# Masking, maximum and shift of the local scores in PSUM, and the sums of v behind the normalisations of the pair before

## What is computed

```python
q_d = q.reshape(B, H, Sd, factor, D).mean(axis=3)      # k_d and v_d likewise; factor 4
out_up = np.repeat(sm_attn(q_d, k_d, v_d), factor, axis=2)
mask = np.abs(pos[:, None] - pos[None, :]) < factor
scores = np.where(mask, scale * np.matmul(q, k.transpose(0, 1, 3, 2)), -1000000000.0)
scores = scores - np.max(scores, axis=-1, keepdims=True)
attn = np.exp(scores)
attn = attn / (np.sum(attn, axis=-1, keepdims=True) + 1e-09)
x = out_up + np.matmul(attn, v)                        # heads side by side: (2304, 512)
h = x @ w_in;  x = np.maximum(0.01 * h, h) @ w_out
h = x @ w_in2; out = (h - np.tanh(h)) @ w_out2
```

## Time and profile before

| what | value |
|---|---|
| median of three runs | 975.33 us |
| lowest, highest | 973.02, 978.2 us |
| the profiled execution: time, span | 974.49, 972.7 us |
| TensorE matmuls busy | 948.7 us (98% of the span) |
| VectorE, ScalarE, GpSimd busy | 553.2, 560.7, 406.8 us |
| chain that ended last: TensorE, GpSimd, ScalarE, VectorE | 82%, 6%, 4%, 2% of the span |

### The profile page before, as it was taken

How to read it: one execution, slowest core, us unless ns; L and a number is a source line. 1 busy time by engine, 2 the same in 40 slices (tenths; PEclk the granted TensorE clock), 3 DMA queues, 4 the chain that set the end, 5 groups by cost and what they waited for, 6 DMA issues and landing times.

```text
span 972.7 us, 19772 instructions
## 1 busy us (share of the span) xinstructions
PE 948.7 (98%) x6960; PEld 889.8 (91%) x6960; DVE 553.2 (57%) x1074; ACT 560.7 (58%) x1355; POOL 406.8 (42%) x343
## 2 busy tenths in 40 slices
PE   6898999999999999999999999999999999999998
PEld 5688999999999999999999989899899899898997
DVE  5853563555445534544334566876676666766764
ACT  4555644645546455445354777775576665766654
POOL 3554823625517337245161847623233233233232
PEclk9979999999999999999999999999999999999999
DMA  6861322112111210212001302100000000000000
GB/s 134 202 193 44 100 51 51 27 25 50 30 39 31 50 31 19 49 27 66 1 2 48 94 24 87 33 34 1 11 22 1 32 0 0 32 0 0 33 1 33
DMA packets 87797, 41.48 MB, mean 43 GB/s; under 512 B 60352, under 2 KB 81344, under 8 KB 87744
## 3 DMA queue, kind: packets, MB, share of 16 engines
q1 hardware_dynamic: 87744, 40.78, 16.0%
HBM read 36.04 MB, written 4.72 MB: 42 GB/s over the span
## 4 chain that ended last, share of the span: by engine, by line
PE 82%; POOL 6%; ACT 4%; issue 3%; DVE 2%; SPq 2%; DMA 1%; POOLq 0%; ACTq 0%; DVEq 0%
PE ph L514 12%; PE ph L515 12%; PE ph L516 12%; PE acc L590 6%; PE acc L591 6%; PE acc L543 6%; PE acc L592 6%; PE acc L544 6%; PE acc L545 6%; PE banks L412 2%; PE banks L431 2%; PE banks L444 2%; POOL in_lo L1071 1%; POOL g_lo L1092 1%; PE banks L405 1%
## 5 line engine op out<-in xcount | busy, mean ns | idle before, releaser
L1092 POOL TENSOR_TENSOR g_lo<-scratch,g_hi 128x384 fp32r<-128x384 f32 x96 | 126.0, 1312 | 257.3 <-ACT g_hi L705 257.1
L940 DVE TENSOR_TENSOR ph<-g,ph 128x288 f32<-128x288 f32 x128 | 59.0, 461 | 165.7 <-ACT g L719 165.1
L514 PE MATMUL ph<-x_hi,w_hi_a 128*128 128x288 f32 (+1 forms) x448 | 144.6, 323 | 0.9 <-DVE g_lo L927 0.7
L515 PE MATMUL ph<-x_lo,w_hi_a 128*128 128x288 f32 (+1 forms) x448 | 140.8, 314 | 0.0
L516 PE MATMUL ph<-x_hi,w_lo_a 128*128 128x288 f32 (+1 forms) x448 | 140.7, 314 | 0.0
L1071 POOL TENSOR_TENSOR in_lo<-w_whole,in_hi 128x512 fp32r<-128x512 f32 x64 | 84.8, 1325 | 131.8 <-ACT in_hi L685 131.8
L719 ACT ACTIVATE g<-ph 128x288 f32<-128x288 f32 x128 | 52.6, 411 | 132.8 <-PE ph L516 132.8
L1076 POOL TENSOR_TENSOR out_lo<-w_whole,out_hi 128x512 fp32r<-128x512 f32 x64 | 86.3, 1348 | 71.9 <-ACT out_hi L689 71.8
L974 DVE SCALAR_TENSOR_TENSOR scratch<-scratch,ph 128x384 f32<-128x384 f32 x96 | 53.2, 554 | 109.7 <-ACT scratch L768 105.1
L767 ACT ACTIVATE scratch<-ph 128x384 f32<-128x384 f32 x96 | 46.8, 488 | 108.3 <-PE ph L516 106.8
L927 DVE TENSOR_TENSOR g_lo<-ph,g_hi 128x288 fp32r<-128x288 f32 x128 | 58.6, 458 | 59.2 <-ACT g_hi L705 59.2
(11 more groups left out here) (265 smaller groups left out, 2681.7 us busy)
## 6 DMA issues: line engine op xcount, KB each, us to landing
out_dram<-o_stage SPq DMA_DIRECT2D x18, 256.0 KB, 2.0
w_whole<-in_moe_w_in_dram SPq DMA_DIRECT2D x16, 256.0 KB, 3.9
w_whole<-in_moe_w_out_dram SPq DMA_DIRECT2D x16, 256.0 KB, 4.4
qn<-in_q_dram SPq DMA_DIRECT2D x26, 144.0 KB
kn<-in_k_dram SPq DMA_DIRECT2D x26, 144.0 KB
v4n<-in_v_dram SPq DMA_DIRECT2D x26, 144.0 KB
vw<-in_v_dram SPq DMA_DIRECT2D x26, 122.5 KB
scratch<-in_moe_w_in_dram SPq DMA_DIRECT2D x8, 256.0 KB, 2.9
```

The lines of the kernel that those rows point to most:

```text
L514: pe.matmul(bank, whi, x_hi[:, c, 0:width], start=(c == 0), stop=False)
L515: pe.matmul(bank, whi, x_lo[:, c, 0:width], start=False, stop=False)
L940: dve.tensor_tensor(ph1[:, f % 2, 0:T1], g1[:, f % 2, :], ph1[:, f % 2, 0:T1], ALU.max)\
L1092: pool.tensor_tensor(g2_lo[:, f % 3, :], g2[:, f % 2, :], g2_hi[:, f % 3, :].bitcast(F32), ALU.subtract).then_inc(g_lo_done, 1)
```

## The change

Two things are changed. In the first batch GpSimd's sums of v move from step 4 to step 6 of a pair; with the stagger of four slots and the order inside a slot they then stand behind step 10 of the pair before. In the twelve later pairs (i > 0) VectorE masks the local scores where they lie in PSUM, takes the maximum of each half from there, and writes `pl` only with the subtraction, for each half by itself. Bank 0 is free after the first half's subtraction, bank 1 after the second's, and ScalarE's exponential waits for the latter. The first four pairs keep the old way. TensorE's instructions are as before.

```diff
+        def first_of(i):
+
+            return isinstance(i, int) and i == 0
...
                 elif step == 7:
-                    act.wait_ge(s.sub_l, i + 1)
+                    if first_of(i):
+                        act.wait_ge(s.sub_l, 1)
+                    else:
+                        act.wait_ge(s.bank_free[1], uses1(i, 3))
                     act.activation(s.pl[:, :, :], s.pl[:, :, :], ACT.Exp, scale=L_SCALE).then_inc(s.exp_l, 1)
...
+            def local_scores(s, bank):
+                n0, n1 = (0, NBA) if bank == 0 else (NBA, NB)
+                return s.banks[:, bank, 0:(n1 - n0) * WIN].rearrange("p (n w) -> p n w", w=WIN)
+
+            def maxima(s, n0, n1):
+                return s.mxl[:, n0:n1].rearrange("p (n o) -> p n o", o=1).to_broadcast([P, n1 - n0, WIN])
...
                 elif step == 4:
                     dve.wait_ge(s.bank_full[0], uses0(i, 3))
-                    src = s.banks[:, 0, 0:NBA * WIN].rearrange("p (n w) -> p n w", w=WIN)
-                    dve.tensor_tensor(s.pl[:, 0:NBA, :], src, band[:, 0:NBA, :], ALU.add).then_inc(s.bank_free[0], 1)
+                    half = local_scores(s, 0)
+                    if first_of(i):
+                        dve.tensor_tensor(s.pl[:, 0:NBA, :], half, band[:, 0:NBA, :], ALU.add)\
+                            .then_inc(s.bank_free[0], 1)
+                    else:
+                        dve.tensor_tensor(half, half, band[:, 0:NBA, :], ALU.add).then_inc(s.masked_half, 1)
                     dve.tensor_reduce(s.kdT[:, :], s.kT[:, PAD:PAD + S].rearrange("p (t f) -> p t f", f=FACTOR),
                                       AX_X, ALU.add).then_inc(s.means_done, 1)
+                    if not first_of(i):
+                        dve.wait_ge(s.masked_half, 2 * i - 1)
+                        dve.tensor_reduce(s.mxl[:, 0:NBA], half, AX_X, ALU.max).then_inc(s.max_half, 1)
...
                 elif step == 5:
                     dve.wait_ge(s.bank_full[1], uses1(i, 3))
-                    src = s.banks[:, 1, 0:(NB - NBA) * WIN].rearrange("p (n w) -> p n w", w=WIN)
-                    dve.tensor_tensor(s.pl[:, NBA:NB, :], src, band[:, NBA:NB, :], ALU.add).then_inc(s.bank_free[1], 1)
-                    dve.wait_ge(s.bank_free[1], uses1(i, 3))
-                    dve.tensor_reduce(s.mxl[:, :], s.pl[:, :, :], AX_X, ALU.max).then_inc(s.max_l, 1)
-                    dve.wait_ge(s.max_l, i + 1)
-                    dve.tensor_tensor(s.pl[:, :, :], s.pl[:, :, :],
-                                      s.mxl[:, :].rearrange("p (n o) -> p n o", o=1).to_broadcast([P, NB, WIN]),
-                                      ALU.subtract).then_inc(s.sub_l, 1)
+                    half = local_scores(s, 1)
+                    dve.tensor_tensor(half, half, band[:, NBA:NB, :], ALU.add).then_inc(s.masked_half, 1)
+                    dve.wait_ge(s.max_half, 2 * i - 1)
+                    dve.tensor_tensor(s.pl[:, 0:NBA, :], local_scores(s, 0), maxima(s, 0, NBA), ALU.subtract)\
+                        .then_inc(s.bank_free[0], 1)
+                    dve.wait_ge(s.masked_half, 2 * i)
+                    dve.tensor_reduce(s.mxl[:, NBA:NB], half, AX_X, ALU.max).then_inc(s.max_half, 1)
+                    dve.wait_ge(s.max_half, 2 * i)
+                    dve.tensor_tensor(s.pl[:, NBA:NB, :], half, maxima(s, NBA, NB), ALU.subtract)\
+                        .then_inc(s.bank_free[1], 1)
...
             def attention(step, s, i):
-                if step == (4 if isinstance(i, int) and i == 0 else 5):
+                if step == (6 if first_of(i) else 5):
```

More of the change, by code:

```diff
@@ L165, in __init__ @@
                 self.v_loaded = sem(f"v_loaded_{which}")
+                self.masked_half, self.max_half = sem(f"masked_half_{which}"), sem(f"max_half_{which}")
                 self.max_l, self.max_d = sem(f"max_l_{which}"), sem(f"max_d_{which}")
@@ L875, in attention @@
                     dve.tensor_reduce(s.kdT[:, :], s.kT[:, PAD:PAD + S].rearrange("p (t f) -> p t f", f=FACTOR),
                                       AX_X, ALU.add).then_inc(s.means_done, 1)
+                    if not first_of(i):
+                        dve.wait_ge(s.masked_half, 2 * i - 1)
+                        dve.tensor_reduce(s.mxl[:, 0:NBA], half, AX_X, ALU.max).then_inc(s.max_half, 1)
+                elif step == 5 and first_of(i):
+                    dve.wait_ge(s.bank_full[1], uses1(i, 3))
+                    dve.tensor_tensor(s.pl[:, NBA:NB, :], local_scores(s, 1), band[:, NBA:NB, :], ALU.add)\
+                        .then_inc(s.bank_free[1], 1)
+                    dve.wait_ge(s.bank_free[1], uses1(i, 3))
+                    dve.tensor_reduce(s.mxl[:, :], s.pl[:, :, :], AX_X, ALU.max).then_inc(s.max_l, 1)
+                    dve.wait_ge(s.max_l, 1)
+                    dve.tensor_tensor(s.pl[:, :, :], s.pl[:, :, :], maxima(s, 0, NB), ALU.subtract)\
+                        .then_inc(s.sub_l, 1)
```

## The result

The changed kernel takes 967.24 us, the median of nine runs (962.71 to 968.43), against 976.53 (972.22 to 981.4) of the kernel before in nine runs beside it. The ratio is 0.9899, 95% interval 0.987 to 0.9929. The forecast was 968.0. Two executions of the kernel before, 981.0 and 981.19 us in one of those series, were in a slower state and are left out of its mean.

What follows compares the result with a forecast made beforehand. TensorE was taken to carry almost the whole 972.7 us span, so only its idle or low-clock time could pay. 974.49 - 2.4 (first batch) - 4.2 (tile 0) + 0 (banks) = 967.9, forecast 968.0 us, range 964.0 to 972.5.

Steps and rivals of the forecast that it cites:

- the forecast's two terms: The gains summed: -2.4 us from GpSimd's order in the first batch, -4.2 us from the subtraction in tile 0.
- The first batch, -2.4 us: A's normalisation no longer waits behind B's v sums on GpSimd; layer one starts 2.4 us earlier, from -1.9 to -3.
- Tile 0, -4.2 us: First pair: subtraction no longer stands behind GpSimd; transposes start 2.9 us earlier, clock gives 0.75 and 0.6; from 0 to -4.9.
- Banks held longer, 0: Later pairs free PSUM banks only after the subtraction; at most 0.1 us in five first pairs; term 0, from +0.5 to -0.5.
- The price of the new instructions: VectorE in later pairs: 0.43 us for 280 elements, 0.51 for 350, a PSUM operand costing nothing extra.
- The clock ahead of layer one: Rival: TensorE's fall to the 1.2 GHz level from 47.8 to 61.4 us doesn't come; time 964 us; 13%.
- my sum: The whole kernel: 974.49 - 2.4 - 4.2 = 967.9 us, forecast 968.0.
- my terms without clock: The first batch's and tile 0's gains, leaving out the 0.75 and 0.6 us expected from tile 0's clock.
- The subtraction doesn't stand behind GpSimd: Rival denied here: in tile 0 the subtraction still stands, only the first term is left, 972.1 us; 10%.
- the first batch's gain was not eaten: Rival denied here: a load of C or D, or D's normalisation behind its v sums, eats it; 970.3 us; 10%.
- PSUM operands cost nothing more: Rival denied here: later pairs' six PSUM instructions cost more than neighbours show; 969.9 us at 0.05 each, 979.4 at 0.22; 7%.

Runs made afterwards that it cites:

- after again: The changed kernel unedited, run once more beside other kernels: 967.09 us, ratio 0.9897 to the kernel before.
- the clock held: Ten dummy transposes of the identity added on TensorE, in the first batch and ahead of layer one; on the changed kernel 962.33 us, on the kernel before 967.46.
- the subtraction late: Kernel before with v sums at step 6 and ten dummy transposes, plus a small extra VectorE maximum ahead of the maximum of tile 0's first pair: 966.12 us.
- the kernel with halves: The changed kernel with masks writing `pl` in SBUF and maxima and subtractions reading it there: 977.09 us; with ten dummy transposes 974.12.
- the order alone: Kernel before with only the first batch's v sums moved to step 6: 967.5 us; with ten dummy transposes 965.67.
- PSUM alone: Changed kernel with the first batch's v sums back at step 4: 970.97 us; with ten dummy transposes 966.5.
- both once more: The changed kernel with the ten dummy transposes, run again beside other kernels on the same chip: 963.46 us, ratio 0.9887 to the kernel before.

## Why the prediction was right, point by point

**The time.** That 968.0 lies so near 967.24 is in part luck. The sum had 6.6 us of gain, counted from 974.49 us; between the medians there are 9.3, counted from 976.53. The gain was put 2.7 us too small and the start 2.0 us too low, and the two nearly cancel. Two profiles that both have the fall of the clock ahead of layer one, before and after again, differ by 7.4 us: 3.20 up to layer one, 0.64 from there to the scores, 3.84 in the stretch, and 0.3 given back behind it. That is the forecast's two terms and 0.8 us more.

**The first batch, -2.4 us.** The mechanism was right, the term a little small: 2.75 us at C's scores as stepped (2.7), but 3.0 at layer one. I had taken 0.3 off for ScalarE's queue; in its place there is a gain of 0.24, since B's normalisation stood behind C's sums as well. I had not looked whether the pattern that I had found for A came again for B.

**Tile 0, -4.2 us, of which 1.35 of clock.** The stretch got shorter by 3.83 us in the profiles (21.37 to 17.54): 2.46 up to the first transpose, where I had 2.9, and 1.37 behind it for the clock, where I had 1.35. With the clock held the standstill costs 2.88 up to the first transpose (16.33 and 13.45, with the subtraction late and without) and nothing behind it; it is longer there because GpSimd's split began 5.58 us behind the scores, in the kernel before 5.17. The remaining wait is 1.11 where I said 0.65: TensorE gets there 12.34 us after the scores (66.22 less 53.88), as stepped (12.38), but ScalarE's weight copy came 0.4 us later than stepped, 8.66 us behind the scores instead of 8.28. What I had not seen is that the standstill need not be there. In the kernel before it was decided by 0.01 us (the expectation of the last kernel says 0.04), and in both profiles with the old subtraction and the clock held it went the other way without any edit to the subtraction. In how many runs of the kernel before it comes is not known, since only one was profiled.

**Banks held longer, 0.** Right: 0.1 us in each later tile, as a gain. The price of the new instructions was right too, 444 to 526 ns against 0.43 to 0.51 us forecast, the mask over 350 elements, which writes in place, being the dearest. By an estimate from the table of the Trainium skill that I had weighed, "VectorE: DVE Perf Modes", section "The TRN2 errata", a PSUM input costs some 65 ns more. The subtraction over 350 elements took 515 ns from SBUF where it did not stand (the minimum in the kernel with halves) and 514 from PSUM. No run here bears it out.

**The clock ahead of layer one, 0 in the sum, a rival with 13% and 964 us.** This is the part that I mis-sized, and in single runs it decides the most. Four of eighteen runs of the changed kernel (962.79, 962.71, 960.52, 962.69) have a clock of 0.999 or 1.0, so that the fall between 48 and 61 us can hardly have come, and the rival describes them; eleven, at 0.992 to 0.994, took 967.1 to 968.5, my sum; three, at 0.995, took 964.2 to 964.9. The forecast of 968.0 hit the second kind. The kernel before had a clock of 0.991 to 0.993 in 27 of 29 runs. With the ten transposes the clock stays up in both, and then, in means, the kernel before takes 968.3 us (on another chip than the next three), the order alone 965.3, PSUM alone 966.6 and both 963.0. So with the clock held the change is worth 5.3 us, about 3 or 3.6 of it the order and 1.7 or 2.3 PSUM. The rest of the 9.8 us between the means (976.08 and 966.26), some 4.5, is what the transposes give the kernel before beyond what they give the changed one. Clock is in it, but not alone: in the profile of the kernel before with the clock held the standstill of tile 0 is gone as well, 2.46 us where it comes. No run here separates the two. For the same reason it is partly luck that my terms without clock (5.25 us) and the 5.3 agree: the first count a standstill that some of the runs behind the second don't have.

**The other rivals.** The subtraction doesn't stand behind GpSimd in any of 24 cases; the first batch's gain was not eaten by `pl_d` or a load; PSUM operands cost nothing more.

What stays open: why the fall comes in one run and not in the next of the same kernel; how the 4.5 us divide; and the long runs at a clock of 1.0, two of 968 us with ten more transposes at the start and three of 970.6 to 972.78 of the kernel before with the clock held.

A version with a lower median than either kernel came out of it, the changed kernel with the ten transposes: 962.33, 963.46 and (with ten more at the start) 962.73 us. Of its 18 runs 16 lie at or below 964.0; of the changed kernel's 18 runs, four. Its ratios to the kernel before (0.9891, 0.9887, 0.9892) lie within the intervals of the changed kernel's, because single runs of the latter are as quick; what it takes away is the longer ones.

## What to carry to other kernels

When an engine that works in order stands for microseconds at an instruction whose operands are ready, look which other engine reads the same memory at that moment, and by how much it was first: a standstill that is decided within 0.1 us can come and go with an edit upstream that has nothing to do with it. Moving one operand to the other memory ends the race whatever the phase is. Once one normalisation is found behind work that isn't due, look for the same pattern at each of its repetitions. And before differences of 2 or 3 us are told from single profiles, hold the clock at one level in both kernels, with a few dummy matmuls in the pauses, and compare them so; but look at the traces too, since such fillers also move the engines against each other, as they did here in tile 0.

## What the hardware showed that I had not expected

- Ten transposes of the identity, in pauses of the first batch, take 4 to 8 us off the median: 967.46 instead of 975.75 us in the kernel before (same series; 968.3 and 974.5 in means), 962.33 and 963.46 instead of 967.09 and 967.24 in the changed one. In the kernel before the granted clock goes from 0.51 to 1.00 between 47.8 and 61.4 us, and the standstill of tile 0 is gone from its profile too. TensorE was busy for 8.42 of the 10 us from 44 to 54 in the kernel before, 9.20 in both once more.
- The two levels are seen in durations where the record's clock shows 1.00 for both: the 36 score matmuls of C took 2.99 us in nine profiles and 1.69 to 2.75 in five others, in the same stretch with a recorded 1.00. There I went by durations.
- Two engines can each be the one that stands, for the same pair of instructions: 1400 instead of 737 ns on GpSimd, or 3.74 instead of 0.81 us on VectorE. VectorE's price is the higher one because GpSimd had a second instruction, of 2.38 us, right behind the first: the subtraction ended 0.67 us behind that.
